# Four pairs of G at a time between the steps of the weight product, each drained by two engines

## What is computed

```python
# attention: B, H, S, Ns, D = 8, 8, 512, 32, 64
a = softmax(x @ state.T / 8);   xread = a @ state          # per batch and head
a2 = softmax(state @ x.T / 8);  sread = a2 @ x
x = concatenate([xread, sread])                            # 4608 tokens x 512
# first feed-forward block, 512 -> 2048 -> 512
h = maximum(x @ w_in, 0);       x = (h * h) @ w_out
# second block, 512 -> 1024 -> 1024 -> 512
return ((x @ w1) * (x @ w2)) @ w3 @ w2_out
```

## Time and profile before

| what | us |
|---|---|
| median of 3 runs (1202.63 to 1203.01) | 1202.88 |
| the profiled execution, its device time | 1202.51 |
| its span in the profile, first to last instruction | 1200.9 |
| TensorE busy, of the span | 1193.2 |
| VectorE busy | 811.5 |
| ScalarE busy | 550.3 |
| GpSimd busy | 103.6 |
| first matmul on zeros | 1.67 |
| first pair of G | 7.75 |
| first late pair | 77.42 |
| first product of the first tile | 88.94 |

### The profile page before, as it was taken

The page is one execution under the profiler, slowest core; times in us unless marked ns, Lnnn a source line. Parts: engine busy times, 40 slices in busy tenths (PEclk is TensorE's granted clock), DMA queues, the critical chain, the costliest instruction groups (busy, mean ns, idle before and its releaser), DMA issues.

```text
span 1200.9 us, 16162 instructions
## 1 busy us (share of the span) xinstructions
PE 1193.2 (99%) x5746; PEld 996.5 (83%) x5746; DVE 811.5 (68%) x1234; ACT 550.3 (46%) x963; POOL 103.6 (9%) x148
## 2 busy tenths in 40 slices
PE   9999999999999999999999999999999999999999
PEld 6687878888888888888888998888888888888888
DVE  6878878677696767868554555785578457754462
ACT  6666655555565555655443342253226223522232
POOL 0001111121121111212000000000000000000000
PEclk9999999999999999999999999999999999999999
DMA  9976664344444444443220438646854784565454
GB/s 328 330 253 242 230 217 146 131 153 158 145 140 150 147 139 147 153 164 124 77 102 22 167 116 311 256 141 228 298 210 175 258 309 167 201 247 193 158 200 168
DMA packets 66014, 225.22 MB, mean 188 GB/s; under 512 B 6432, under 2 KB 10016, under 8 KB 57760
## 3 DMA queue, kind: packets, MB, share of 16 engines
q1 hardware_dynamic: 50800, 171.46, 40.3%
q0 software_dynamic: 15152, 52.96, 12.6%
HBM read 162.53 MB, written 61.87 MB: 187 GB/s over the span
## 4 chain that ended last, share of the span: by engine, by line
PE 97%; DVE 1%; DMA 0%; ACT 0%; issue 0%; SPq 0%; DVEq 0%; ACTq 0%
PE ps_y L810 55%; PE ps_h L810 27%; PE ps_t L810 13%; PE ps_h L872 1%; PE ps_t L835 1%; PE ps_y L872 0%; DMA raw<-in_moe_w_out 0%; PE ps_t L872 0%; DVE v_lo L1428 0%; DVE t L1518 0%; DVE X_lo L1428 0%; SPq L612 0%; DVE stage L1536 0%; ACT v_hi L1128 0%; SPq L606 0%
## 5 line engine op out<-in xcount | busy, mean ns | idle before, releaser
L810 PE MATMUL ps_y<-v_hi,X_hi 128*128 128x512 f32 (+1 forms) x576 | 219.0, 380 | 0.3 <-DVE v_lo L1428 0.3
L810 PE MATMUL ps_y<-v_hi,X_lo 128*128 128x512 f32 (+1 forms) x576 | 217.6, 378 | 0.0
L810 PE MATMUL ps_y<-v_lo,X_hi 128*128 128x512 f32 (+1 forms) x576 | 217.6, 378 | 0.0
L1428 DVE TENSOR_TENSOR t<-t 128x512 f32<-128x512 f32 (+1 forms) x144 | 94.8, 658 | 93.4 <-ACT t L1226 92.8
L1226 ACT ACTIVATE t<-ps_h 128x512 f32<-128x512 f32 (+1 forms) x144 | 82.7, 574 | 151.6 <-PE ps_h L810 151.0
L1128 ACT CAST v_hi<-t 128x512 fp32r<-128x512 f32 (+1 forms) x144 | 86.1, 598 | 120.5 <-DVE t L1428 117.8
L810 PE MATMUL ps_y<-X_hi,s_odd 128*128 128x512 f32 x448 | 140.6, 389 | 0.0
L1428 DVE TENSOR_TENSOR v_lo<-t,v_hi 128x512 fp32r<-128x512 f32 (+1 forms) x144 | 95.4, 662 | 60.7 <-ACT v_hi L1128 50.3
L810 PEld LDWEIGHTS ps_y<-v_hi,X_lo 128*128 128x128 f32 x576 | 108.4, 188 | 20.3
L810 PEld LDWEIGHTS ps_y<-v_hi,X_hi 128*128 128x128 f32 x576 | 108.5, 188 | 20.2 <-issue 0.7
L810 PEld LDWEIGHTS ps_y<-v_lo,X_hi 128*128 128x128 f32 x576 | 108.5, 188 | 19.3
(11 more groups left out here) (239 smaller groups left out, 2310.2 us busy)
## 6 DMA issues: line engine op xcount, KB each, us to landing
top<-s_scratch SPq DMA_DIRECT2D x16, 1792.0 KB, 7.3
s_odd<-s_scratch SPq DMA_DIRECT2D x16, 1792.0 KB, 7.3
GA<-w_scratch SPq DMA_DIRECT2D x19, 1024.0 KB, 5.2
raw<-g_scratch SPq DMA_DIRECT2D x64, 256.0 KB
GB<-w_scratch SPq DMA_DIRECT2D x9, 1024.0 KB, 5.3
raw<-in_moe_w_in SPq DMA_DIRECT2D x32, 256.0 KB
raw<-in_x_T SPq DMA_DIRECT2D x32, 256.0 KB
raw<-in_x_tok SPq DMA_DIRECT2D x32, 256.0 KB
```

The costliest lines, as they stand in the source:

```text
L810: mm = nc.tensor.matmul(dst, w, m, start=first and n == 0, stop=last and n == 2, skip_group_check=onto)
L1428: return nc.vector.tensor_tensor(dst, a, b, op)
```

## The change

The list is written anew. Pairs come in groups of four, behind steps 4, 9 and 12; the last four of the 16 join the late ones, which makes 20 of them. The splits of the w3T and wout2 pieces are two steps ahead of the step that needs them rather than one, the pieces of w_in come later, and the list begins with the pieces of steps 0 and 1, not with the state and w_in. Attention slots 3 and following are put beside other steps. Within the groups a pair uses `ps_h` and `ps_t` in turn and waits for the pair two before it. Each pair is drained by both engines, ScalarE the first bank and VectorE the second. The state is loaded behind the first six pieces. There are 10 matmuls on zeros.

```diff
--- before.py
+++ after.py
@@ -52,7 +52,7 @@
     KF = DF // P
     KM = DM // P
     KG = DF2 // P
-    WARM = 18
+    WARM = 10
     RAW_AT = 4736
     TOP_AT = 214144
     X_AT = 21120
@@ -405,22 +405,31 @@
         N_PAIRS = PAIRS * BG * Q
         STEPS = N_PAIRS // BG
 
-        def step_pieces(k):
-
-            return ([("piece", "w_in", k)] + ([("piece", "wout2", k)] if k < KG else []) + [("piece", "w3T", k)])
-
-        beside = {1: [("att", 0)], 3: [("piece", "xT", 0, 0), ("piece", "xT", 1, 0)],
-                  4: [("piece", "xT", 2, 0), ("piece", "xT", 3, 0)], 5: [("att", 3)], 6: [("att", 4)], 7: [("att", 5)],
-                  8: [("att", 6)], 9: [("att", 7), ("piece", "x", 0, 0)], 10: [("att", 8), ("piece", "x", 1, 0)],
-                  11: [("att", 9), ("att", 10), ("piece", "x", 2, 0)], 12: [("att", 11), ("piece", "x", 3, 0)],
-                  13: [("att", 12), ("piece", "G", 0, 0)], 14: [("att", 13), ("piece", "G", 1, 0)],
-                  15: [("piece", "G", 2, 0), ("piece", "G", 3, 0)]}
-        order = [("st", 0)] + step_pieces(0)
+        GROUP = 4
+        LEAD = 2
+        group_after = {4: 0, 9: 1, 12: 2}
+
+        def w3_pieces(k):
+
+            return ([("piece", "wout2", k)] if k < KG else []) + [("piece", "w3T", k)]
+
+        w_in_of = {1: [0], 2: [1], 3: [2], 4: [3], 7: [4], 8: [5, 6], 9: [7], 10: [8], 11: [9, 10], 12: [11], 13: [12],
+                   14: [13], 15: [14, 15]}
+        others = {2: [("st", 0), ("st", 1), ("st", 2)], 3: [("att", 0)],
+                  5: [("piece", "xT", 0, 0), ("piece", "xT", 1, 0)], 6: [("piece", "xT", 2, 0), ("piece", "xT", 3, 0)],
+                  10: [("piece", "x", 0, 0)], 11: [("piece", "x", 1, 0)], 12: [("piece", "x", 2, 0)],
+                  13: [("piece", "x", 3, 0), ("piece", "G", 0, 0)], 14: [("piece", "G", 1, 0), ("piece", "G", 2, 0)],
+                  15: [("piece", "G", 3, 0)]}
+        beside = {6: [3], 7: [4], 8: [5], 9: [6, 7], 10: [8], 11: [9, 10], 12: [11], 13: [12], 14: [13], 15: [15]}
+        order = w3_pieces(0) + w3_pieces(1)
         for k in range(STEPS):
-            order += step_pieces(k + 1) if k + 1 < STEPS else []
-            order += [("st", k + 1)] if k < 2 else []
-            order += [("pair", k), ("wp", k)] + beside.get(k, [])
-        order += [("att", 15)] + [("pair", p) for p in range(STEPS, N_PAIRS)] + [("piece", "wout", 0)]
+            order += w3_pieces(k + LEAD) if k + LEAD < STEPS else []
+            order += [("piece", "w_in", j) for j in w_in_of.get(k, [])] + others.get(k, [])
+            order += [("wp", k)] + [("att", u) for u in beside.get(k, [])]
+            if k in group_after:
+                order += [("pair", GROUP * group_after[k] + n) for n in range(GROUP)]
+        GROUPED = GROUP * len(group_after)
+        order += [("pair", p) for p in range(GROUPED, N_PAIRS)] + [("piece", "wout", 0)]
 
         def row_of(p):
 
@@ -432,20 +441,17 @@
 
         def pair_banks(p):
 
-            return ps_h[:] if p < STEPS else (ps_h[:], ps_y[:, 0:2], ps_y[:, 2:4], ps_t[:])[p % 4]
+            return (ps_h[:], ps_t[:])[p % 2] if p < GROUPED else (ps_h[:], ps_y[:, 0:2], ps_y[:, 2:4], ps_t[:])[p % 4]
 
         def last_in_banks(p):
 
-            return p - 1 if p <= STEPS else p - 4 if p >= STEPS + 4 else -1
-
-        def drainer(p):
-
-            return p % 2
+            return p - 2 if p <= GROUPED else p - 4 if p >= GROUPED + 4 else -1
 
         def wait_drained(eng, p):
 
             if p >= 0:
-                eng.wait_ge(g_drained[drainer(p)], len([q for q in range(p + 1) if drainer(q) == drainer(p)]))
+                for drained in g_drained:
+                    eng.wait_ge(drained, p + 1)
 
         def buffer_of(p):
 
@@ -620,7 +626,6 @@
                             sp.dma_start(dst, A_block(i, kk, row, col)).then_inc(A_loaded, 16)
 
             early = start_pieces + flat(tile0_slots)
-            load_st(0)
             def wait_G(piece):
 
                 for p in (last_pair(piece) - 1, last_pair(piece)):
@@ -638,9 +643,9 @@
                         wait_G(early[r])
                     load_piece(r, early[r])
                     r += 1
-                    if r == 3:
-                        load_st(1)
-                        load_st(2)
+                    if r == 6:
+                        for part in range(3):
+                            load_st(part)
             for r in range(r, R_1):
                 if early[r][0] == "G":
                     wait_G(early[r])
@@ -856,10 +861,13 @@
                 c, bg, q = pair_of(p)
                 if p < 3:
                     pe.wait_ge(st_split, p + 1)
-                if p == STEPS + 1:
+                if p == GROUP + 1:
+                    pe.wait_ge(att_free[0], uses(0, 0))
+                    pe.wait_ge(att_free[1], uses(0, 1))
+                if p == GROUPED + 1:
                     for drained in wp_drained:
                         pe.wait_ge(drained, 4)
-                if p == STEPS + 3:
+                if p == GROUPED + 3:
                     pe.wait_ge(att_free[0], uses(0, 4))
                     pe.wait_ge(att_free[1], uses(0, 3))
                 pe.wait_ge(piece_split, number["w_in", row_of(p)] + 1)
@@ -887,8 +895,11 @@
 
             for what in order:
                 if what[0] == "att":
+                    if what[1] == 3:
+                        wait_drained(pe, GROUP - 1)
                     if what[1] == 12:
                         pe.wait_ge(ident_ready, 1)
+                        wait_drained(pe, GROUPED - 1)
                     attention_slot(what[1], 0, [number["xT", k, 0] + 1 for k in (1, 3)], number["x", R - 1, 0] + 1)
                 if what[0] == "pair":
                     g_pair(what[1])
@@ -1177,7 +1188,7 @@
                 if p < STEPS:
                     wait_for(act, g_stored[buffer_of(p)], stored(buffer_of(p), p))
                 act.wait_ge(g_full, p + 1)
-                copy(drained_to(p), pair_banks(p)).then_inc(g_drained[0], 1)
+                copy(drained_to(p)[:, 0, :], pair_banks(p)[:, 0, :]).then_inc(g_drained[0], 1)
 
             for what in order:
                 if what[0] == "st":
@@ -1190,14 +1201,14 @@
                     attention_slot(what[1], 0, 0)
                 if what[0] == "piece":
                     kind, k = what[1:3]
-                    if kind == "w3T" and k >= 4:
-                        act.wait_ge(wp_full, k - 3)
+                    if kind == "w3T" and k >= 3:
+                        act.wait_ge(wp_full, max(k - 3, 1))
                     if kind == "G":
                         act.wait_ge(wp_full, KG + k + 1)
                     if kind == "wout":
                         act.wait_ge(g_full, N_PAIRS - 6 + k + 1)
                     split_piece(number[what[1:]], what[1:], 0)
-                if what[0] == "pair" and drainer(what[1]) == 0:
+                if what[0] == "pair":
                     drain_pair(what[1])
                 if what[0] == "wp" and what[1] % KG == KG - 1:
                     act.wait_ge(wp_full, what[1] + 1)
@@ -1510,12 +1521,12 @@
 
 
             def drain_pair(p):
-                if p == N_PAIRS - 1:
+                if p == N_PAIRS - 2:
                     dve.wait_ge(wp_stored, 16 * 2)
                 if p < STEPS:
                     wait_for(dve, g_stored[buffer_of(p)], stored(buffer_of(p), p))
                 dve.wait_ge(g_full, p + 1)
-                nc.vector.tensor_copy(drained_to(p), pair_banks(p)).then_inc(g_drained[1], 1)
+                nc.vector.tensor_copy(drained_to(p)[:, 1, :], pair_banks(p)[:, 1, :]).then_inc(g_drained[1], 1)
 
             for what in order:
                 if what[0] == "st":
@@ -1527,7 +1538,7 @@
                     attention_slot(what[1], 0, 0)
                 if what[0] == "piece":
                     split_piece(number[what[1:]], what[1:], 0)
-                if what[0] == "pair" and drainer(what[1]) == 1:
+                if what[0] == "pair":
                     drain_pair(what[1])
                 if what[0] == "wp" and what[1] % KG == KG - 1:
                     dve.wait_ge(wp_full, what[1] + 1)
```

## The result

The changed kernel takes 1206.20 us, median of 17 runs (1203.25 to 1208.77), against 1203.32 for the kernel before on the same chips, also of 17 (1202.44 to 1205.97). The ratio is 1.0023, 95% interval [1.0016, 1.0030]: slower by 0.23%, by a little more than the 0.2% that the prediction took for no change (the interval reaches to both sides of it), and 4.6 us above the forecast. The profiled execution took 1206.96 us, its span is 1205.4. Not only the median has moved: single runs of the changed kernel lie 5.5 us apart, and 16 of the 17 of the kernel before within 1.3 us.

What follows compares the result with a forecast made beforehand. TensorE was taken as the bound, 97% of the chain of waits. Terms -1.35 - 5.5 - 1.4 + 0.45 + 2.9 + 3.75 + 0.2 gave -0.95, from 1202.51 to 1201.6 us; range 1196.5 to 1205.

Steps and rivals of the forecast that it cites:

- no change: Whole kernel: a difference under 0.2%, 2.4 us; this outcome was given 0.57.
- Start: First step of the weight product at 6.4, where the first pair stood at 7.75: 1.35 us gained.
- Switching: TensorE's change from 128 rows to 64 and back, 0.42 each, paid 3 times instead of 16: 5.5 us less.
- The two waits of the drains: TensorE waits 2.8 us before pair 6 for ScalarE's drain, 3.65 before pair 10 for VectorE's; with restart 2.9 and 3.75.
- DMA and the queues: Up to slot 15, 82 units of 256 KB done at about 66 against 73.8, so hidden; nothing taken for it.
- a load comes late behind the stores: Rival: a group stores 2 MB at once, 6 us; w3T 11 or 13 landing 3 us late gives 1204.6; chance 0.07.
- the second rival: The clock falls to 1.2 GHz in the two long waits: one fall gives 1203.5, both 1205.3; chance 0.10.
- Its mark: Sign of the clock's fall: the second matmul behind a wait comes 0.43 later and not 0.23.
- Nothing behind 88 us: From the first tile on nothing is touched; no gain or loss expected there.
- The forecast first product: First product of the first tile, expected near 88, where the first tile started at 88.94 before.

Runs made afterwards that it cites:

- the kernel with the clock kept up: Changed kernel with third-group stores behind the w_in 15 and G 3 loads, G 3 split behind late pairs, pairs 5 and 9 made four times: 1201.23 us.
- both repairs: Changed kernel with third-group stores behind the loads of w_in 15 and G 3, and G 3 split behind the late pairs; not run with nothing added.
- the one-part kernel: Kernel before, with each pair drained by both engines, ScalarE the first bank and VectorE the second, nothing else: 1205.15 us, ratio 1.0015.
- the first experiment: Changed kernel with the matmuls of pairs 5 and 9 made four times over, no new result: 1206.91 us, ratio 1.0031.
- the groups ahead: Changed kernel with the groups of steps 9 and 12 listed ahead of attention slots 6, 7 and 11: 1206.47 us; also combined with other edits.
- G 3 late: Changed kernel with G 3 split behind the late pairs instead of before step 15's stage copies: 1202.82 us, ratio 0.9998.
- both gains: Changed kernel with stores behind loads, G 3 behind late pairs, groups two and three drained by ScalarE alone, pair 5 made five times: 1202.00 us.
- tile loads held back: Changed kernel with the first tile's loads issued only after the loop over the list: 1205.36 us, ratio 1.0016.

## Why the prediction was wrong

The direction and the size of the sum were off: 1201.6 was forecast, with 1196.5 to 1205.0 as range and "no change" as the likeliest, and 1206.20 came. Point by point:

- **Start.** Forecast 6.4, measured 6.18. But in this trace the clock was still low: the first passes of real work cost 0.42 until about 7.6 us, where in the kernel before the pitch was 0.23 from about 5.6 on the earlier trace rows. The five steps that followed ran until 20.78 rather than 20.2. These 0.6 us belong to the execution and not to the ten matmuls: in the second trace of the same kernel the first step starts at 5.93 at full pitch and the first group at 19.80.
- **Switching.** As forecast; the steps between groups follow at 0.228.
- **The two waits of the drains.** Right in place, releaser and size: 2.56 for 2.8, 2.87 for 3.65, pair 6 0.4 us late and pair 10 1.3. The queues of ScalarE and VectorE, followed with durations of the trace before, were worth the trouble. The second wait came later since pair 7 was drained at 48.4 and not 47.0: TensorE was at half its clock just before. In the second trace, where it was not, the waits are 2.64 and 3.41, and pair 10 starts at 59.16, forecast 59.75.
- **DMA and the queues: the step that failed.** "So it hides, by less than before" and "I take nothing for it". I had counted units, 82 of them until about 66 us, and found room; I had also written down that eight pieces are under way ahead of the stores. What I did not do is ask which pieces these are. The last two of the list, w_in 15 and G 3, were not among them: they are issued right behind the four stores of the third group, and the stage copies stand behind their splits. The wait before pair 13 was 2.20 us with a fall of the clock behind it that cost 1.3 more, and moving the stores or the split of G 3 gave 3.1 or 3.4 us back, which brings the time into the stated range. The rival "a load comes late behind the stores" named this mechanism at 0.07 and 1204.6, with w3T 11 or 13 as the late piece.
- **The clock, left out of the sum.** It was the second rival, at 0.10, and it happened. Its mark was put down beforehand: the second matmul behind a wait comes 0.43 later. By the letter the mark failed, for behind pairs 6 and 10 that distance is 0.31; the 0.43 comes from the third pass on behind pair 6, and from the sixth on behind pair 10. Whoever looked at the second matmul alone would have missed both falls. By the Trainium skill, "TensorE: Matmul & The Clock Gate", section on HAM oscillation, idle gaps bring the low clock back, and the trace agrees, with 0.50 granted from 46 to 48 us behind a gap of 2.56; but the second trace has a gap of 2.64 with no fall behind it. A sum that has two waits of 3 us in it should hold their falls as a term. What it is worth can be read across the 17 runs of the changed kernel, the same program each time:

| mean granted clock of a run | runs | median us |
|---|---|---|
| 0.999 | 6 | 1204.05 |
| 0.997 | 4 | 1206.51 |
| 0.996 | 5 | 1206.96 |
| 0.994 | 2 | 1208.55 |

  The ends of this table are 4.5 us apart. A clock lower by 0.005 over 1205 us would be worth 6.0 us by my estimate, enough to account for it. It is a correlation and not all of the spread: the six runs at 0.999 lie from 1203.25 to 1205.59 themselves. In the kernel repaired for its loads, one fall cost 1.5 us between two traces, and the kernel with the clock kept up is 1.2 to 1.9 us below its neighbours.
- **Nothing behind 88 us.** Off by 0.84 us in favour of the change in this pair of traces, at the entry into the tile loop, where the profile shows no engine that TensorE waits for. The other versions differ there by as much among themselves, so this is no effect of the change that the runs show. I made no experiment on it.

The forecast first product, 88.0, and the measured one, 94.28, are 6.3 apart. Pair 12 is 2.6 late (0.6 from the start, the rest from the slow passes behind the waits), pair 13 another 2.4 from the loads, and from there to the first product it is 14.7 instead of 13.4, 1.3 for the eight slow passes. In the second trace, with a quick start and two falls instead of three, the first product comes at 92.04.

What the change was worth without its accident: with the stores moved, 1203.11 against 1203.16 for the kernel before beside it; in that form the forecast of no change holds, by the forecast's own reasons, and what is left between its first product (90.24) and the forecast one (88.0) is mostly the clock. The fastest version of the study is the repaired one with the clock kept up, 1201.23, 0.15% below the kernel before; the same drained by ScalarE, without idle work, 1201.66.

What stays open: whether VectorE's amount of work or the chain through ScalarE and back sets the wait before pair 10 (two experiments moved that wait and none took it away); what both repairs give with nothing else; and why the clock falls behind a wait in one execution and not in the next.

## What to carry to other kernels

When an order of work is changed, list for each queue which transfer is issued last before a burst and which first behind it, and what stands behind that one on the engine that splits it; a ledger of bytes cannot see it. When a change merges many short waits into a few long ones, price the clock behind each long one; the work saved may be less than the passes that then run slow. Banks that two engines drain come back with the later of them, so share a drain only where both stand ready.

## What the runs showed of the hardware

- The clock's fall behind a wait is not certain. In the 15 traces of the changed order and of the one-part kernel, it did not fall behind any of TensorE's waits up to 1.38 us (0.65 and 1.38 in the first experiment, 1.24 to 1.35 with the groups ahead). It fell behind waits of 1.82, 1.95, 2.20, 2.56, 2.87 and 2.98 to 3.21 us and behind every one from 3.39 up, but stayed at 1.00 behind 2.09 (G 3 late), 2.31 (both gains), 2.64 (the second trace) and 3.38 (tile loads held back). The changed kernel had mean clocks from 0.994 to 0.999 and times 5.5 us apart.
- The fall can come when TensorE is already at work again: behind the wait of 2.87 us five passes went at full pitch, and the first at 0.43 started 1.2 us after the restart.
- The low stretch is longer behind a longer wait: about eight 512-column passes behind 2.2 to 2.9 us, a clock of 0.50 from 58 to 64 us around and behind a wait of 4.60.
- A 256 KB load issued right behind 2 MB of stores was split 8 to 11 us later, with the DMA engines at about full share (0.97 to 1.05 from 64 to 76 us); issued just ahead of them it took under 7. Loads issued later seem to cost it 0.5 to 1.7 us more, by one trace against five.
- The windows of the first 8 us read a granted clock of 1.00 although the matmuls there come every 0.43 us; the pitch of the matmuls told the level where that column didn't. When the pitch falls to 0.23 differs between executions of the same start: about 7.6 us in the first trace of the changed kernel, about 6 us in the second.
